# Attention scores of the ninth to the last head pair as three fp32r products of high and low halves, split by GpSimd

## The reference

```python
# q, k, v: (4 batches, 12 heads, 448 positions, 64) float32; q and k are drawn eight times as large as v
scores = q @ k.T / sqrt(64);  scores = cap * tanh(scores / cap)      # cap = 30
attn = exp(scores - max) / (sum(exp(scores - max)) + 1e-9)
x = (attn @ v), heads side by side                                   # 1792 tokens x 768
g = s * relu(x @ w_in) ** 2 + b                                      # w_in 768 x 2048
y = g @ w_out                                                        # w_out 2048 x 768
```

## Time and profile before

| | us |
|---|---|
| median of 3 runs (658.07 to 3653.71) | 658.17 |
| the profiled execution's time | 658.21 |
| its span, first to last instruction | 656.4 |
| TensorE busy | 644.7 |
| VectorE busy | 339.0 |
| ScalarE busy | 247.2 |
| GpSimd busy | 36.7 |

### The profile page before, as it was taken

One profiled execution on the slowest core, in us unless ns is written; L12 is line 12 of the kernel. 1 busy time (PEld: TensorE's weight loads), 2 busy tenths in 40 slices (PEclk: granted clock), 3 DMA queues, 4 the chain that ended last, 5 costly groups with the idle time before them and its releaser, 6 DMA issues.

```text
span 656.4 us, 7953 instructions
## 1 busy us (share of the span) xinstructions
PE 644.7 (98%) x3098; PEld 494.9 (75%) x3098; DVE 339.0 (52%) x611; ACT 247.2 (38%) x255; POOL 36.7 (6%) x32
## 2 busy tenths in 40 slices
PE   7999999999999999999999999999999999999998
PEld 4333666666666666666667999999999999999997
DVE  2798977798666666676676423322332121113111
ACT  5777444444444444444440323222322121213110
POOL 2331321210000000000000000000000000000000
PEclk9999999999999999999999999999999999999999
DMA  7543143324222222222111411123152233215002
GB/s 217 169 145 108 37 123 119 106 76 132 86 87 73 86 87 72 87 87 72 57 43 42 159 48 49 49 72 109 43 191 62 57 128 90 64 28 183 1 0 85
DMA packets 38101, 57.94 MB, mean 88 GB/s; under 512 B 11440, under 2 KB 29872, under 8 KB 38064
## 3 DMA queue, kind: packets, MB, share of 16 engines
q1 hardware_dynamic: 37632, 57.43, 28.0%
q10 hardware_dynamic: 432, 0.00, 0.0%
HBM read 40.90 MB, written 16.52 MB: 87 GB/s over the span
## 4 chain that ended last, share of the span: by engine, by line
PE 94%; DVE 4%; ACT 1%; issue 1%; DVEq 0%
PE hid L320 13%; PE hid L322 12%; PE hid L321 12%; PE pv L291 9%; PE scores L334 8%; PE scores L335 8%; PE scores L336 8%; PE scores L262 5%; PE pv L334 4%; PE pv L335 4%; PE pv L336 4%; PE scores L274 3%; PE scores L271 2%; PE pv L344 1%; DVE e_sum L490 1%; DVE e_sum L486 1%
## 5 line engine op out<-in xcount | busy, mean ns | idle before, releaser
L320 PE MATMUL hid<-x_hi,w_hi 128*128 128x448 f32 x384 | 143.9, 375 | 0.3 <-DVE xt L539 0.3
L322 PE MATMUL hid<-x_hi,w_lo 128*128 128x448 f32 x384 | 140.3, 365 | 0.0
L321 PE MATMUL hid<-x_lo,w_hi 128*128 128x448 f32 x384 | 140.2, 365 | 0.0
L320 PEld LDWEIGHTS hid<-x_hi,w_hi 128*128 128x128 f32 x384 | 72.1, 188 | 29.3 <-issue 23.1
L334 PE MATMUL scores<-x_hi,w_hi 128*128 128x448 f32 x256 | 93.5, 365 | 0.0
L335 PE MATMUL scores<-x_lo,w_hi 128*128 128x448 f32 x256 | 93.5, 365 | 0.0
L336 PE MATMUL scores<-x_hi,w_lo 128*128 128x448 f32 x256 | 93.5, 365 | 0.0
L557 DVE SCALAR_TENSOR_TENSOR x_lo<-e,const,x_hi 128x448 fp32r<-128x448 f32 x48 | 32.1, 683 | 103.8 <-ACT x_hi L410 103.8
L396 ACT ACTIVATE e<-e,const 128x1792 f32<-128x1792 f32 (+1 forms) x48 | 77.0, 1604 | 1.6
L322 PEld LDWEIGHTS hid<-x_hi,w_lo 128*128 128x128 f32 x384 | 72.1, 188 | 5.7
L321 PEld LDWEIGHTS hid<-x_lo,w_hi 128*128 128x128 f32 x384 | 72.2, 188 | 5.2
(11 more groups left out here) (67 smaller groups left out, 721.3 us busy)
## 6 DMA issues: line engine op xcount, KB each, us to landing
qk<-q_k SPq DMA_DIRECT2D x24, 448.0 KB, 3.3
hidden_scratch<-hidden_sb SPq DMA_DIRECT2D x48, 224.0 KB, 2.0
e<-hidden_scratch SPq DMA_DIRECT2D x48, 224.0 KB, 2.8
work<-w_in SPq DMA_DIRECT2D x24, 256.0 KB, 4.1
e<-w_out SPq DMA_DIRECT2D x16, 384.0 KB, 3.1
y_t<-qk SPq DMA_DIRECT2D x24, 224.0 KB, 2.0
v_sb<-v SPq DMA_DIRECT2D x24, 192.0 KB, 2.4
k_ab<-q_k SPq DMA_DIRECT2D x48, 16.0 KB, 3.0
```

The lines of the kernel that those rows point to most:

```text
L320: nc.tensor.matmul(out, w_hi[:, j, w], x_hi[:, batch % 2, c, :], start=c == 0, stop=False)
L321: nc.tensor.matmul(out, w_hi[:, j, w], x_lo[:, batch % 2, c, :], start=False, stop=False)
L322: last = nc.tensor.matmul(out, w_lo[:, j, w], x_hi[:, batch % 2, c, :], start=False, stop=c == CT - 1)
```

## The change

For pairs 8 to 23 (`SPLIT = PAIRS + 2`), GpSimd splits q and k as they arrive: a copy of the 128x896 tile to fp32r, a subtraction for the low half, and four copies of 64x64 that put the key rests into block diagonal tiles for each half. The halves have two slots. TensorE then computes each score tile as three fp32r matmuls, with the two heads' matmuls (64 rows each) alternating. The key rests of these pairs are no longer loaded by DMA. GpSimd's list becomes: low halves of pieces 0 to 14, split of pair 8, pieces 15 to 17, split of pair 9, pieces 18 to 20, split of pair 10, pieces 21 to 23, splits of pairs 11 to 23. The copy, the subtraction and the four small copies each wait for the one before.

```diff
+SPLIT = PAIRS + 2
...
             def load_qk(p):
...
-                reach(sp, scores_done, 2 * (p - QK_SLOTS + 1))
+
+                if p - QK_SLOTS < SPLIT:
+                    reach(sp, scores_done, 2 * (p - QK_SLOTS + 1))
+                else:
+                    sp.wait_ge(qk_lo_done, p - QK_SLOTS + 1 - SPLIT)
                 sp.dma_start(qk[:, i].rearrange("p a n -> p (a n)"), q_k[batch, c]).then_inc(qk_in[i], 16)
-                sp.dma_start(k_ab[0:D, i, 0:D], q_k[batch, c, 0:D, S + FULL * P:]).then_inc(qk_in[i], 16)
-                sp.dma_start(k_ab[D:P, i, D:P], q_k[batch, c, D:P, S + FULL * P:]).then_inc(qk_in[i], 16)
+                if p < SPLIT:
+                    sp.dma_start(k_ab[0:D, i, 0:D], q_k[batch, c, 0:D, S + FULL * P:]).then_inc(k_ab_in[i], 16)
+                    sp.dma_start(k_ab[D:P, i, D:P], q_k[batch, c, D:P, S + FULL * P:]).then_inc(k_ab_in[i], 16)
...
+            def split_product(out, n, k_hi, k_lo, q_hi, q_lo):
+
+                return nc.tensor.matmul(out, k_lo if n == 2 else k_hi, q_lo if n == 1 else q_hi,
+                                        start=n == 0, stop=n == 2)
+
+            def first_split_scores(p):
+                i = p % 2
+                pe.wait_ge(qk_hi_done, p - SPLIT + 1)
+                pe.wait_ge(qk_lo_done, p - SPLIT + 1)
+
+                pe.wait_ge(tanh_done, 2 * p)
+                for t in range(FULL - 1):
+                    keys = slice(t * P, (t + 1) * P)
+                    for n in range(3):
+                        for head in range(2):
+                            rows = slice(head * D, (head + 1) * D)
+                            last = split_product(scores[:, 2 * t + head, 0:S], n, qk_hi[rows, i, 1, keys],
+                                                 qk_lo[rows, i, 1, keys], qk_hi[rows, i, 0, :], qk_lo[rows, i, 0, :])
+                last.then_inc(scores_done, 1)
+
+            def last_split_scores(p):
+                i = p % 2
+                pe.wait_ge(tanh_done, 2 * p + 1)
+                pe.wait_ge(k_ab_done, 4 * (p - SPLIT + 1))
+                for n in range(3):
+                    split_product(scores[:, 2, 0:S], n, k_ab_hi[:, i, :], k_ab_lo[:, i, :],
+                                  qk_hi[:, i, 0, :], qk_lo[:, i, 0, :])
+                keys = slice((FULL - 1) * P, FULL * P)
+                for n in range(3):
+                    for head in range(2):
...
                 last.then_inc(scores_done, 1)
...
             for p in range(PAIRS, ALL):
                 batch, c = divmod(p, PAIRS)
-                if p + 1 < ALL:
+                if p + 1 < SPLIT:
                     first_scores(p + 1)
+                elif p + 1 < ALL:
+                    first_split_scores(p + 1)
...
+            def split_qk(p):
+                raw, i, done = p % QK_SLOTS, p % 2, p - SPLIT
+                flat = "p a n -> p (a n)"
+                pool.wait_ge(qk_in[raw], 16 * (p // QK_SLOTS + 1))
+
+                if p - 2 >= SPLIT:
+                    pool.wait_ge(scores_done, 2 * (p - 1))
+                nc.gpsimd.tensor_copy(qk_hi[:, i].rearrange(flat), qk[:, raw].rearrange(flat)).then_inc(qk_hi_done, 1)
+                pool.wait_ge(qk_hi_done, done + 1)
+                nc.gpsimd.tensor_tensor(qk_lo[:, i].rearrange(flat), qk[:, raw].rearrange(flat),
+                                        qk_hi[:, i].rearrange(flat).bitcast(F32), ALU.subtract).then_inc(qk_lo_done, 1)
+                pool.wait_ge(qk_lo_done, done + 1)
+                for head in range(2):
+                    rows = slice(head * D, (head + 1) * D)
+                    nc.gpsimd.tensor_copy(k_ab_hi[rows, i, rows], qk_hi[rows, i, 1, FULL * P:]).then_inc(k_ab_done, 1)
+                    nc.gpsimd.tensor_copy(k_ab_lo[rows, i, rows], qk_lo[rows, i, 1, FULL * P:]).then_inc(k_ab_done, 1)
...
-            for piece in range(PIECES):
...
+            for piece in range(15):
+                w_in_low(piece)
+            for p in range(SPLIT, ALL):
+                split_qk(p)
+                first = 15 + 3 * (p - SPLIT)
+                for piece in range(first, min(first + 3, PIECES)):
+                    w_in_low(piece)
```

More of the change, by code:

```diff
@@ L63, in attention_ffn @@
         k_ab = sb("k_ab", [P, QK_SLOTS, P], F32)
+        qk_hi = sb("qk_hi", [P, 2, 2, S], F32R)
+        qk_lo = sb("qk_lo", [P, 2, 2, S], F32R)
+        k_ab_hi = sb("k_ab_hi", [P, 2, P], F32R)
+        k_ab_lo = sb("k_ab_lo", [P, 2, P], F32R)
         v_sb = sb("v_sb", [P, QK_SLOTS, VT * D], F32)
@@ L100, in attention_ffn @@
         zeros_ready = sem("zeros_ready")
+        split_zeros = sem("split_zeros")
+        qk_hi_done = sem("qk_hi_done")
+        qk_lo_done = sem("qk_lo_done")
+        k_ab_done = sem("k_ab_done")
         qk_in = [sem(f"qk_in{i}") for i in range(QK_SLOTS)]
+        k_ab_in = [sem(f"k_ab_in{i}") for i in range(QK_SLOTS)]
         v_in = [sem(f"v_in{i}") for i in range(QK_SLOTS)]
@@ L255, in first_scores @@
                 i = p % QK_SLOTS
-                pe.wait_ge(qk_in[i], 48 * (p // QK_SLOTS + 1))
+                pe.wait_ge(qk_in[i], 16 * (p // QK_SLOTS + 1))
                 reach(pe, tanh_done, 2 * p)
@@ L268, in last_scores @@
                 pe.wait_ge(tanh_done, 2 * p + 1)
+                pe.wait_ge(k_ab_in[i], 32 * (p // QK_SLOTS + 1))
                 if p == 0:
@@ L275, in last_scores @@
                                             qk[rows, i, 0, :], start=True, stop=True)
+                last.then_inc(scores_done, 1)
[14 more added lines that the diff above has]
+                                                 qk_lo[rows, i, 1, keys], qk_hi[rows, i, 0, :], qk_lo[rows, i, 0, :])
+                last.then_inc(scores_done, 1)
+            def last_split_scores(p):
[9 more added lines that the diff above has]
+                        rows = slice(head * D, (head + 1) * D)
+                        last = split_product(scores[:, head, 0:S], n, qk_hi[rows, i, 1, keys],
+                                             qk_lo[rows, i, 1, keys], qk_hi[rows, i, 0, :], qk_lo[rows, i, 0, :])
                 last.then_inc(scores_done, 1)
@@ L354, in _ @@
                 batch, c = divmod(p, PAIRS)
-                if p + 1 < ALL:
+                if p + 1 < SPLIT:
                     first_scores(p + 1)
+                elif p + 1 < ALL:
+                    first_split_scores(p + 1)
                 for chunk in range(SHARE * c, SHARE * c + 8):
                     hidden_chunk(batch - 1, chunk)
-                if p + 1 < ALL:
+                if p + 1 < SPLIT:
                     last_scores(p + 1)
+                elif p + 1 < ALL:
+                    last_split_scores(p + 1)
                 values(p)
@@ L626, in _, with w_in_low @@
         def _(pool):
+            def w_in_low(piece):
+                f, c = divmod(piece, CT)
+                of = slice(f * JPP, (f + 1) * JPP), slice(c * P, (c + 1) * P)
+                pool.wait_ge(w_in_hi, piece + 1)
+                nc.gpsimd.tensor_tensor(w_lo[:, of[0], of[1]], work[:, piece % 4, :].rearrange("p (j n) -> p j n", n=P),
+                                        w_hi[:, of[0], of[1]].bitcast(F32), ALU.subtract).then_inc(w_in_lo, 1)
+            def split_qk(p):
[10 more added lines that the diff above has]
+                for head in range(2):
+                    rows = slice(head * D, (head + 1) * D)
+                    nc.gpsimd.tensor_copy(k_ab_hi[rows, i, rows], qk_hi[rows, i, 1, FULL * P:]).then_inc(k_ab_done, 1)
+                    nc.gpsimd.tensor_copy(k_ab_lo[rows, i, rows], qk_lo[rows, i, 1, FULL * P:]).then_inc(k_ab_done, 1)
+                pool.wait_ge(k_ab_done, 4 * (done + 1))
             n = 2 * FULL * D
@@ L632, in _ @@
             pool.wait_ge(zeros_ready, 4)
-            for piece in range(PIECES):
[L634 to L638, removed]
+            for half in (k_ab_hi, k_ab_lo):
+                nc.gpsimd.memset(half[0:D, :, D:P].bitcast(F32), 0.0).then_inc(split_zeros, 1)
+                nc.gpsimd.memset(half[D:P, :, 0:D].bitcast(F32), 0.0).then_inc(split_zeros, 1)
+            pool.wait_ge(split_zeros, 4)
+            for piece in range(15):
[5 more added lines that the diff above has]
+                    w_in_low(piece)
 def kernel(q, k, v, cap, moe_w_in, moe_w_out, moe_s, moe_b):
@@ L659 @@
     }
-    nc = bacc.Bacc("TRN2", target_bir_lowering=False, num_devices=1)
+    nc = bacc.Bacc("TRN2", target_bir_lowering=False, num_devices=1,
+                   dynamic_dma_scratch_size=2048)
     ins = [nc.dram_tensor(name, a.shape, mybir.dt.from_np(a.dtype), kind="ExternalInput").ap()
```

## The result

The changed kernel takes 666.61 us (median of 4 runs, 665.33 to 668.75) against 658.12 of the kernel before: ratio 1.0129, 95% interval [1.0109, 1.0148]. It is 8.5 us slower, 1.3%; 667 was predicted, and the spans differ by the same 8.5 (664.9 and 656.4).

What follows compares the result with a forecast made beforehand. TensorE was taken to bound the kernel, busy 98% of the span. Waits put pair 11's step 16.4 us late, 13 pairs give 7.3 back: +9.1 on the 656.4 span, plus 1.8 around it, 667 us; range 657 to 682.

Steps and rivals of the forecast that it cites:

- the single waits: TensorE idle ahead of the first split products of pairs 8 to 11: 4.3, 4.3, 4.8 and 4.8 us.
- TensorE's gain: Scores in fp32r instead of float32 save TensorE 0.56 us a pair, giving steps of 16.13 us.
- That rival: Row tiles do worse in fp32r: heads one after the other, 691 us, or weight loads laid bare, 680; chance 0.11 for both.
- S: Time from GpSimd being free to both split halves being there: 4.2 us, bounds 2.9 and 6.3.
- C: VectorE's time lost per split by taking turns with GpSimd, lengthening the chain of pieces: 3.0 us, bounds 1.9 and 4.8.
- Where TensorE waits: TensorE waits for splits behind pieces at pairs 8 to 11, none from 12; the step with pair 11 starts 16.4 us late.
- the rival on the clock: TensorE's clock falls to 1.2 GHz in the waits; only the last counts, 2.4 us, about 670; chance 0.2 inside the forecast's range.
- The sum: 16.4 us late at pair 11 less 7.3 us back over 13 pairs: +9.1 us on the span of 656.4.
- In the steps p = 7 to 9 TensorE is later by more than VectorE is, so that slack grows: Later squares, hidden stores and ScalarE's rectifying do not hold TensorE in these steps.
- the whole gain, 649.2: Rival of no lasting wait: GpSimd's halves come in time, turns cost nothing, 9.0 us kept, 649.2 us; chance 0.12.
- VectorE becomes the bound: Rival: with C at 4.8 VectorE needs 17.1 us a step against 16.1, so 675 to 688 us; chance 0.13.

Runs made afterwards that it cites:

- e3_split_unused: Changed kernel, but scores of all pairs are the float32 ones and TensorE does not wait for the splits GpSimd still makes; 665.65 us, ratio 1.0102.
- e2_from_13th: Changed kernel with split scores only from pair 12 on, GpSimd doing all 24 pieces before its first split; 650.64 us, ratio 0.9876.
- e4_aligned: Changed kernel with each split one group of pieces earlier and held until VectorE's transpose of the sums of pair p - 2; 657.53 us, ratio 0.9979.
- e9_early_piece: Changed kernel with SyncE loading pieces 17, 20 and 23 ahead of the hidden stores of the step before; 662.06 us, ratio 1.0057.
- e5_copy_twice: Changed kernel with GpSimd's copy of q and k made twice in each split; 669.11 us, ratio 1.0165.
- e1_splits_first: Changed kernel with only GpSimd's list changed, each split one group of pieces earlier; 658.21 us, ratio 0.9996.
- e6_kept_busy: Changed kernel with TensorE multiplying w_hi by x_hi, result overwritten, while it waits for the halves of pairs 8 to 11; 665.93 us, ratio 1.0111.

## Why the prediction was right

The time lies within the stated range, within 2% of the time before, and the cause is the one forecast: four waits for splits that stand behind pieces. One step inside it failed, the length of the single waits; and that 667 met 666.6 so closely is partly luck, as the sum below shows.

**TensorE's gain, 0.56 us a pair.** Right to the last digit that the view shows: groups of 1.42 and 1.42 us for a forecast of 1.43 and 0.61 + 0.81, steps of 16.13. The two heads do run at once in fp32r; a slot is 0.20 us. That rival is dead. The sentence of the Trainium skill (TensorE: Matmul & The Clock Gate, The mechanism) that a weight load overlaps matmuls in flight only where its row group differs does not hold here: loads of the same row group stay hidden at 0.20 us a slot. The same section also lets a load go ahead into a background weight buffer; with that the trace would agree, though no run here shows the buffer.

**S, 4.2 us.** From GpSimd being free to both halves: 85.17 - 80.97 = 4.2, then 3.8, 4.2 and 4.2. The copy takes 0.93 us alone (0.8 assumed), the subtraction 2.1 (2.1 assumed), and the waits for VectorE's operations make up the rest.

**C, 3.0 us.** The low half of pieces 17, 20 and 23 ends at 100.96, 122.01 and 142.22, for 98.90, 116.81 and 134.65 before; with the 0.49 us that this trace is ahead at piece 12 (76.10 for 76.59, most of it the shorter opening), the lag is 2.6, 5.7 and 8.1: C was 2.6, 3.1 and 2.4. It was somewhat over-sized, 0.9 us over the three. The taking of turns was read rightly from two rows: L542 and L546 beside the split took 4.83 us instead of 2.36.

**Where TensorE waits.** At all four pairs and none after, and the step with pair 11 starts at 146.48, 15.0 us later than before, 15.5 with the trace's offset, for 16.4 forecast; the 0.9 is C's. But the forecast of the single waits (4.3, 4.3, 4.8, 4.8) failed: they are 4.36, 0.76, 5.31 and 1.45. What fills most of the difference is the rival on the clock. After the waits of 4.36 and 5.31 us the granted clock is 0.50 of full speed, 1.2 GHz, for 5.7 us each, so that TensorE comes 2.6 us later to the next wait (18.74 and 18.77 us of work in those steps for 16.18 in the one between), and that wait is shorter by as much. The forecast gave this 0.2, and 2.4 us for the last wait; the last wait was short, the clock stayed at 1.00 behind it, and so it cost nothing. Keeping TensorE busy showed it: full clock, 0.7 us.

**The sum.** The spans count from the same start, so it is 15.0 that stands against 16.4. From there to VectorE's last copy of the output (653.33 before, 661.24 after) 7.1 us come back for 7.3, since the first step takes 16.29 us. What follows that copy, where no scores are left, is 0.6 us longer (3.7 for 3.1), and why is open. 15.0 - 7.1 + 0.6 = 8.5. So the forecast was 1.4 too high at pair 11 (C, and the shorter opening), 0.2 too generous behind it, and knew nothing of the last 0.6; these offset each other to 0.6.

**What it missed.** "In the steps p = 7 to 9 TensorE is later by more than VectorE is, so that slack grows" is true of this kernel and was the reason for pricing VectorE's lag at nothing. It was not said what the lag costs when TensorE is not late: e3_split_unused has 7.4 us, through square, store, the three slots of hidden tiles and the rectifying. That is also why the whole gain, 649.2, was not simply one reordering away. The rival "VectorE becomes the bound" stood for late steps and was wrong there (e2_from_13th runs its steps at the full gain of 0.56), but VectorE is the bound of steps 7 to 10 once the first wait is taken out. Of two engines that are both late, the later one hid the other.

The view shows which VectorE operations take turns. In a late step L602 (two inputs from SBUF, 0.63 us alone) meets the copy and takes 1.30, so the one-input copy costs VectorE too. The reduction L569 runs beside the subtraction and stays at 1.08, while in another step a scalar addition of 28 columns, L572, took 1.18 for 0.23 and ended with the subtraction beside it:

```profile
165.00 2.13 POOL L699 TENSOR_TENSOR qk_lo<-qk,qk_hi 128x896 fp32r<-128x896 f32 x1
165.97 1.18 DVE L572 TENSOR_SCALAR quads<-parts,const 32x28 f32<-32x28 f32 x1
...
241.56 0.93 POOL L697 CAST qk_hi<-qk 128x896 fp32r<-128x896 f32 x1 [12.75 <-DMA qk<-q_k]
241.67 1.30 DVE L602 TENSOR_TENSOR x_lo<-xt,x_hi 128x448 fp32r<-128x448 f32 x1
242.57 2.38 POOL L699 TENSOR_TENSOR qk_lo<-qk,qk_hi 128x896 fp32r<-128x896 f32 x1
...
244.03 1.08 DVE L569 TENSOR_REDUCE parts<-turned 128x28 f32<-128x896 f32 x1
```

The Trainium skill (SBUF — State Buffer, Who interferes with whom) has this as one lock on ports shared by the two engines, held for a whole instruction, which VectorE needs for two SBUF inputs or a mode that uses both ports, and not for a reduction. The trace agrees in these rows: L602 is of the first kind, L569 of the last. That L572 is of the second kind is inferred from its wait. It is what e4_aligned ran into: L572 took 2.1 us there in each split.

## What to carry to other kernels

An engine's share of the span does not tell whether it has time: read the end of its last instruction ahead of the new work against the moment the result is wanted, step by step. Work given to GpSimd can be paid for by VectorE: here its operations with two inputs from SBUF waited, and so did one scalar operation of 28 columns. So give GpSimd its work in steps in which VectorE has room; here starting at pair 12, with 12 pairs instead of 16, turned +8.5 us into -7.6, of which 0.9 in the trace is the shorter opening. And when a wait is removed, look at once for the engine that was late behind it.

## What the runs showed of the hardware that was not expected

The length of a wait of TensorE did not by itself decide whether the granted clock fell. It fell to 0.50 during the waits of 4.36 and 5.31 us of the changed kernel and stayed at 1.00 after ones of 2.24 and 2.43 (e9_early_piece). But it also fell 0.4 us behind a wait of 2.61 (e5_copy_twice), 0.4 us behind one of 4.21 (e1_splits_first) and 1.1 us behind one of 2.92 (e3_split_unused), and did not fall after one of 2.79 in that same run. The waits of 2.61 and 4.21, and what followed (from the windows view: us, busy times, clock, DMA):

```profile
104.00:106.50 2.50, 0.01 (x1) 0.00 (x0) 2.47 (x2) 0.00 (x0) 2.50 (x1) 1.00 0.14 52
107.10:110.00 2.90, 2.90 (x13) 2.27 (x11) 2.80 (x5) 1.06 (x1) 1.06 (x3) 0.50 0.03 6
...
135.60:139.80 4.20, 0.00 (x0) 0.00 (x0) 2.76 (x7) 0.59 (x2) 1.57 (x2) 1.00 0.39 127
140.20:143.60 3.40, 3.40 (x11) 3.05 (x10) 1.83 (x3) 3.37 (x3) 1.90 (x2) 0.50 0.76 218
```

Low stretches lasted from 3.4 us (e1_splits_first) to some 7 us (e4_aligned). In the changed kernel two of 5.7 us of work each cost the program 0.7 us by e6_kept_busy, because a later wait took the rest up.
